# First step of a fused attention and feed-forward kernel: when the first weights are loaded, who assembles the scores, who fills x's gaps, and in what pieces GpSimd works

## The reference

```python
for t in range(S):                       # S = 768
    cur = einsum('bhd,bhe->bhde', u[None] * kt, vt)
    y[:, :, t] = einsum('bhd,bhde->bhe', rt, state + cur)
    state = wt[:, :, :, None] * state + einsum('bhd,bhe->bhde', kt, vt)
x = y.transpose(0, 2, 1, 3).reshape(3072, 384)
h = x @ w_in;  x = where(h > 0, h, exp(min(h, 0)) - 1) @ w_out      # first layer
h = x @ w_in2; x = (h * sigmoid(1.702 * h)) @ w_out2                # second layer
```

## Time and profile before

| | |
|---|---|
| median of 3 runs | 989.51 us (989.06 to 989.93) |
| the profiled execution's own time | 990.9 us |
| its span | 988.7 us |
| PE busy | 943.1 us, 95% of the span |
| PE weight loads busy | 916.1 us, 93% |
| DVE busy | 554.5 us, 56% |
| ACT busy | 457.9 us, 46% |
| POOL busy | 73.0 us, 7% |
| PE in the chain that ended last | 94% |

### The profile page before, as it was taken

The page is one execution under the profiler, slowest core; times in us unless marked ns, Lnnn a source line. Parts: engine busy times, 40 slices in busy tenths (PEclk is TensorE's granted clock), DMA queues, the critical chain, the costliest instruction groups (busy, mean ns, idle before and its releaser), DMA issues.

```text
span 988.7 us, 27078 instructions
## 1 busy us (share of the span) xinstructions
PE 943.1 (95%) x11872; PEld 916.1 (93%) x11872; DVE 554.5 (56%) x910; ACT 457.9 (46%) x875; POOL 73.0 (7%) x66
## 2 busy tenths in 40 slices
PE   3678999999999999999999999999999999999998
PEld 3568999999889999999999999999999999999998
DVE  7899576586676675766853434343433343434333
ACT  3445645636437446455464764333333333333332
POOL 1055000000000000000000542000000000000000
PEclk9979999999999999999999999999999999999999
DMA  7361131221211402212003620000000000000000
GB/s 206 80 170 34 37 94 26 56 51 25 58 50 26 103 3 59 71 26 56 27 2 116 258 81 1 25 1 24 0 18 7 5 19 0 24 1 25 1 25 25
DMA packets 15734, 47.30 MB, mean 48 GB/s; under 512 B 2864, under 2 KB 6832, under 8 KB 15632
## 3 DMA queue, kind: packets, MB, share of 16 engines
q1 hardware_dynamic: 13600, 40.50, 14.7%
q0 software_dynamic: 1552, 4.84, 1.8%
q10 hardware_dynamic: 480, 0.40, 0.2%
HBM read 35.71 MB, written 8.85 MB: 45 GB/s over the span
## 4 chain that ended last, share of the span: by engine, by line
PE 94%; issue 3%; DVE 2%; DMA 1%; ACT 0%; SPq 0%; POOL 0%; DVEq 0%; ACTq 0%; POOLq 0%
PE psum L1214 42%; PE psum L1227 41%; PE psum L1004 4%; PE psum L1114 2%; PE psum L966 1%; PE psum L1109 1%; PE psum L1082 1%; PE psum L1047 1%; PE psum L1040 1%; DMA arena<-w_channels_dram 0%; DVE arena L673 0%; DVE blocks L727 0%; ACT blocks L413 0%; DVE arena L667 0%; PE psum L1013 0%
## 5 line engine op out<-in xcount | busy, mean ns | idle before, releaser
L1214 PE MATMUL psum<-x_hi,w_split 128*128 128x384 f32 x1536 | 395.1, 338 | 0.7 <-issue 0.6
L1227 PE MATMUL psum<-g_hi,w_split 128*128 128x384 f32 x1536 | 393.0, 337 | 0.0
L1214 PEld LDWEIGHTS psum<-x_hi,w_split 128*128 128x128 f32 x1536 | 281.1, 188 | 1.2 <-issue 1.1
L1227 PEld LDWEIGHTS psum<-g_hi,w_split 128*128 128x128 f32 x1536 | 278.5, 189 | 0.4 <-issue 0.3
L1214 PE MATMUL psum<-x_lo,w_split 128*128 128x384 f32 x768 | 263.5, 343 | 5.1 <-DVE x_lo L757 4.1
L1227 PE MATMUL psum<-g_lo,w_split 128*128 128x384 f32 x768 | 262.2, 341 | 0.1
L472 ACT ACTIVATE g_hi<-gate 128x384 fp32r<-128x384 f32 x256 | 134.5, 525 | 178.6 <-DVE gate L776 96.1
L781 DVE TENSOR_TENSOR g_lo<-gate,g_hi 128x384 fp32r<-128x384 f32 x256 | 150.1, 586 | 117.9 <-ACT g_hi L472 117.7
L774 DVE TENSOR_TENSOR gate<-expo,psum 128x384 f32<-128x384 f32 x128 | 70.8, 554 | 162.6 <-ACT expo L468 162.6
L1214 PEld LDWEIGHTS psum<-x_lo,w_split 128*128 128x128 f32 x768 | 144.6, 188 | 6.5 <-issue 4.2
L1227 PEld LDWEIGHTS psum<-g_lo,w_split 128*128 128x128 f32 x768 | 144.9, 189 | 2.9 <-issue 0.6
(11 more groups left out here) (86 smaller groups left out, 458.3 us busy)
## 6 DMA issues: line engine op xcount, KB each, us to landing
v_sb<-v_tokens_dram SPq DMA_DIRECT2D x8, 576.0 KB, 6.2
arena<-w_channels_dram SPq DMA_DIRECT2D x14, 288.0 KB, 5.0
arena<-k_channels_dram SPq DMA_DIRECT2D x14, 288.0 KB, 4.4
arena<-r_channels_dram SPq DMA_DIRECT2D x14, 288.0 KB, 4.9
x_scratch<-x_sb SPq DMA_DIRECT2D x7, 576.0 KB, 3.2
arena<-x_scratch SPq DMA_DIRECT2D x1, 4032.0 KB, 12.5
staging<-weights_dram SPq DMA_DIRECT2D x9, 384.0 KB, 3.6
blocks<-weights_dram SPq DMA_DIRECT2D x9, 384.0 KB, 4.0
```

Source lines behind the costliest of these rows:

```text
L1214: mm = pe.matmul(hidden(f), w_tile(f, lo, m * P), xx, start=n == 0, stop=n == 3 * KT - 1)
L1227: mm = pe.matmul(acc(to, m), w_tile(f, lo, (KT + m) * P), gg, start=f == 0 and n == 0, stop=f == NF - 1 and n == 2)
```

## The change

The change touches the first step and the weights' split.

1. SP no longer issues v, the identity and the five first weight slices behind the inputs. It waits for DVE's updates of the first pair of heads: slices 0, 1 and the identity after level 1, slice 2 after level 2, slice 3 and v after level 3, slice 4 after level 4. The load of the next step's w waits for level 5 of both pairs (before: level 1).
2. DVE does level 1's update of the first pair after two of six products of the tree instead of after all six.
3. The fourth strip of scores is assembled by DVE (`first_assemble`), the other three by ACT. PE's third group of transposes takes bank 0 again and waits for ACT's first copy; the wait for the first pick moves on to the key-value products.
4. Of the six gap DMAs, SP issues two (four before), ACT two as before, POOL two.
5. DVE's low halves: slices 0 and 1 no longer stand between the picks and the states; slice 5 goes to POOL (11 slices there), and slice 4 comes after x's split. ACT's high halves of slices 5 to 15 are issued later, two slices nearer to their use.
6. DVE does the last five products of step 1's tree after the update of level 1, and no longer ahead of the first gate.
7. POOL's low half is four instructions of 192 columns and no longer one of 768.

```diff
@@ turn_banks, gaps_filled @@
-            return (FIRST[0], FIRST[1], FIRST[2]) if is_first(i) else (Z, X, Y)
+            return (FIRST[0], FIRST[1], FIRST[0]) if is_first(i) else (Z, X, Y)
...
                 engine.wait_ge(gap_first, 32)
-                engine.wait_ge(gap_low, 64)
-            else:
-                engine.wait_ge(gap_low, i * 48 + 64)
-                engine.wait_ge(gap_high, i * 48)
+            engine.wait_ge(gap_low, i * 48 + 32)
+            engine.wait_ge(gap_high, i * 48 + 32)
@@ SyncE @@
-                            sp.wait_ge(upd_first[pair], 1)
+                            sp.wait_ge(upd_first[pair], 5)
...
-                        sp.dma_start(x_raw[112:128, 2, :], y3[96:112, 0, :]).then_inc(gap_low, 16)
...
-                    for m in range(KT):
+                    for m in range(2 if is_first(i) else KT):
...
-                sp.dma_start(v_sb[:].rearrange("p c u a e -> p (c u a e)"), v_dram[0]).then_inc(v_in, 16)
-                sp.dma_start(ident[:, :], ident_dram).then_inc(ident_in, 16)
-                for f in range(NW1):
-                    sp.dma_start(w1_raw[f], weights1[f]).then_inc(w1_first[f], 16)
+                for level, fs in ((1, (0, 1)), (2, (2,)), (3, (3,)), (4, (4,))):
+                    sp.wait_ge(upd_first[0], level)
+                    for f in fs:
+                        sp.dma_start(w1_raw[f], weights1[f]).then_inc(w1_first[f], 16)
+                    if level == 1:
+                        sp.dma_start(ident[:, :], ident_dram).then_inc(ident_in, 16)
+                    if level == 3:
+                        sp.dma_start(v_sb[:].rearrange("p c u a e -> p (c u a e)"), v_dram[0]).then_inc(v_in, 16)
@@ GpSimd @@
-                    at = 2 * f * WF
-                    pool.tensor_tensor(w_split[:, at + WF:at + 2 * WF], w1_raw[w1_place(f)],
-                                       w_split[:, at:at + WF].bitcast(F32), ALU.subtract).then_inc(wlo_done, 1)
-
-                for f in range(NW1, 8):
+                    at, n = 2 * f * WF, WF // 4
+                    for z in range(4):
+                        low = pool.tensor_tensor(w_split[:, at + WF + z * n:at + WF + (z + 1) * n],
+                                                 w1_raw[w1_place(f)][:, z * n:(z + 1) * n],
+                                                 w_split[:, at + z * n:at + (z + 1) * n].bitcast(F32), ALU.subtract)
+                    low.then_inc(wlo_done, 1)
+
+                pool.wait_ge(wlo_done, 1)
+                load(5)
+                pool.wait_ge(y3c_first, 1)
+                pool.wait_ge(y3d_first, 1)
+                pool.dma_start(x_raw[48:64, 2, :], y3[32:48, 0, :]).then_inc(gap_high, 16)
+                pool.dma_start(x_raw[112:128, 2, :], y3[96:112, 0, :]).then_inc(gap_high, 16)
+                for f in range(6, 8):
                     pool.wait_ge(wlo_done, f - NW1 + 1)
                     load(f)
-                pool.wait_ge(wlo_done, 6)
-                load(8)
-                for f in range(6, NF):
+                pool.wait_ge(wlo_done, NW1)
+                for f in range(NW1, NF):
                     w1_low(f)
@@ ScalarE @@
-                        after = {2: 10, 3: 11, 4: 12, 5: 13, 6: 14, 7: 15}
+                        after = {2: 8, 3: 9, 4: 10, 5: 11, 6: 12, 7: 13, 8: 14, 9: 15}
...
                     off32(i, 1)
+                    higher(8)
                     whole(g, 9 + s)
+                    higher(9)
...
-                for j in range(4):
+                for j in range(3):
                     assemble(0, j)
-                w1_high(5)
-                w1_high(6)
                 act.wait_ge(y3_first, 2)
...
-                w1_high(7)
                 first_split()
                 for u in range(U):
                     bonus(1, u)
+                w1_high(5)
                 act.wait_ge(wlo_done, NW1)
                 whole(0, 0)
-                w1_high(8)
+                w1_high(6)
                 whole(0, 1)
-                w1_high(9)
+                w1_high(7)
@@ VectorE @@
+                def first_assemble(j):
+
+                    dve.wait_ge(pick_done, N_PICK)
+                    o = 32 * j
+                    t = 32 * (j % 2)
+                    dve.tensor_copy(scores[o:o + 32, :, :, :, t:t + 32].rearrange("p u c a t -> p (u c a) t"),
+                                    diag[o:o + 32, :].rearrange("p (g t) -> p g t", t=32)).then_inc(asm_done, 1)
...
-                for m in range(6):
+                for m in range(2):
                     tree_pair(m, 0)
-                for k in range(1, 3):
-                    grow_pair(k, 0)
+                grow_pair(1, 0)
+                for m in range(2, 6):
+                    tree_pair(m, 0)
+                grow_pair(2, 0)
...
-                for f in range(2):
-                    w1_low(f)
+                first_assemble(3)
                 states(0, 0, 0, range(6))
-                w1_low(2)
+                w1_low(0)
                 dve.wait_ge(y3_first, 2)
                 dve.tensor_copy(*y3_first_view(1)).then_inc(y3d_first, 1)
-                for f in range(3, 5):
+                for f in range(1, 4):
                     w1_low(f)
...
                 first_split()
-                w1_low(5)
-                for m in range(1, 6):
-                    tree(1, m)
+                w1_low(4)
                 gated(0, 0)
...
                 grow_k(1, 1)
+                for m in range(1, 6):
+                    tree(1, m)
                 step(0, 1, 1, 0, 0)
@@ TensorE @@
                         if n == 8:
-                            pe.wait_ge(pick_done, PICKS[1])
+                            pe.wait_ge(kt_done, 1)
...
                     pe.wait_ge(kt_done, i * N_KT + N_KT)
+                    if is_first(i):
+                        pe.wait_ge(pick_done, PICKS[1])
                     pe.sem_inc(level_open, 1)
```

## The result

| | before | after |
|---|---|---|
| median, measured side by side | 990.36 us (18 runs) | 994.44 us (18 runs, 990.9 to 997.7) |
| ratio after / before | | 1.0039, 95% interval 1.0027 to 1.0050 |
| profiled execution, span | 990.9, 988.7 us | 994.93, 992.8 us |
| POOL busy | 73.0 us | 89.5 us |

The change makes the kernel 4 us slower, not 6 us faster: 10 us off, with the wrong sign. Up to 100 us the walk of the prediction is nearly that of the trace. The loss comes right behind it, from 101 to 126 us.

The account below looks back on a forecast made before the run. PE bounds from 400 us on, PE and DVE share 66 to 100 us, and waits through DVE, ACT and DMAs lie ahead. Gains 1.9 + 4.1 = 6.0 us; median 983.5 us, range 979.5 to 988.0.

Parts of the forecast that it names:

- Loads level by level: Start to about 37 us: later weight loads free PE's instruction fetch; 3.06 us gained, 1.2 given back, net 1.9 us.
- The second stop: PE's 0.66 us stop 256 passes after the one near 14 us, read as an instruction wait with DMAs idle.
- the first stop's price: PE's 2.17 us stop near 14 us: DMA traffic was said to delay its instruction block by about 3.2 us.
- Assemble: First step's scores: ACT does three of four strips, so PE's outputs come 0.86 us earlier.
- Gaps: Split of x: two gap DMAs per queue, last landing about 49.4 us; PE's first `up` gains 0.48 us.
- First gate, tree, levels 1 to 4: Step 1: gate follows exp at once, level 1 2.2 us earlier, level 3 only 1.2, level 4 3.3 us.
- POOL in quarters: 66 to 100 us: DVE needs 5.5 us, not 7.9, from level 3 to 4; 4.1 us gained at 100 us.
- POOL starves: Rival, chance 0.06: quarters wait for DVE, slices take 8.9 us, ACT and PE wait for weights; 993.3 us.
- What would show it wrong: PE stopping as long at a later block, or ACT waiting for staging buffers between 65 and 100 us.

Follow-up runs that it names:

- the quarters and the later order: Kernel before, with POOL's low half in four pieces and ACT's high halves of slices 8 to 15 two units later: 984.75 us, 0.9946.
- k held: Changed kernel, with SP holding its load of k until slice 15 has landed: 990.24 us, 1.0004 against the kernel before.
- slice 15 alone moved: Changed kernel, with ACT's high half of slice 15 behind the key copies and slice 10's gate: 988.91 us, 1.0005 against the kernel before.

## Why the prediction was wrong

- **Loads level by level:** right in kind; right in size because two terms that were both too large cancel (3.06 - 1.2 forecast, 2.45 - 0.59 in the trace). 1.9 us forecast, 1.85 in the trace (last pick done at 36.90 and not 38.75 us), 1.8 alone. The second stop, from which the price of the first was taken, was not at idle DMAs: the earlier trace rows shows 22 to 22.5 us, but from 21.0, where the request was put, to 21.5 the DMA engines were busy 0.93 of the time, as this row of the kernel before shows (its last three numbers are clock, DMA share and GB/s):

```profile
21.00:21.50 0.50, 0.50 (x48) 0.50 (x41) 0.50 (x1) 0.00 (x0) 0.00 (x0) 1.00 0.93 184
```

  So the 3.2 us of the first stop's price have no undisturbed row to stand on. The Trainium skill, "Runtime: NRT & Kernel Launch", section "Instruction fetch mechanics", calls such a crossing "mostly hidden"; the 2.17 us that went with the loads say that it isn't under 16 busy DMA engines, and this case's trace disagrees with the page at the next stop too (0.66 us before, 1.25 after).
- **Assemble:** right (0.86 forecast, 0.87 measured on ACT), but not seen in the time of the kernel that has it.
- **Gaps:** wrong in size. I counted queues and let the DMAs land at their old pace (2.5 to 2.9 us in the profile before); with slice loads, r and v around them they take 4.1 to 4.7 us. The split waits 3.02 us, and the first `up` starts at 50.96 us, 0.9 us sooner than before, where 1.9 + 0.48 = 2.4 were forecast.
- **First gate, tree, levels 1 to 4:** right in the mechanism. The gate follows its exp at once, the tree costs what it should. With the 1.9 us of the loads in it the forecast had PE ahead by 4.1 us at level 1, 3.1 at level 3, 5.2 at level 4 and 6.0 at 100 us; the trace has 2.3, 2.6, 4.7, and 5.2 at the transposes (95.04 us). What the gaps took is mostly won back by level 4. Two slips in the working change nothing: 66.8 + 3.9 + 0.8 is 71.5 and not 71.3 us, and the lower bound of the loads' gain is 3.06 - 3.2 = -0.1 and not -0.2 us.
- **The step that failed is "POOL in quarters".** It priced the quarters by what DVE gains and let the 4.1 us at 100 us stand to the end ("Whatever PE gains there it keeps, since PE is dense behind"). That DVE gains is right: with the quarters alone PE is 3.0 us ahead at the transposes (97.22 and not 100.24 us), and the kernel is 4.7 us faster. What was put at nothing is what stands behind them, the wait of ACT for slice 15 with the key copies behind it: 4.05 us of PE standing still at 101 us, 3.4 us of half clock, and about 1.8 us of a second stretch at half clock. What the quarters cost POOL (5.3 us per slice) I had written down only as the rival "POOL starves", with a 0.06 chance, "from 7.2 us per slice on". Its mechanism is the right one: ACT, in order, waits for weights, and PE behind it. Its threshold was wrong for three reasons that the runs show. ACT's high halves stood two units later, so that POOL's later slices began later: load(15) goes out at 86.40 us with the quarters alone, at 97.49 with the quarters and the later order, at 96.29 in the changed kernel. I took 4.4 us for a load; beside k's it took 6.6 (k held: 3.7 us, 1.0004). And I priced PE's stop at its own length, without the stretch at half clock behind it, 3.4 us.
- **What would show it wrong** was named: "ACT is seen waiting for staging buffers between 65 and 100 us". It is, for 1.30 us up to 94.14 and from 97.2 us on. POOL's slices were to stay under 5 us; the longest takes 5.29. The change lists the high halves that move on ACT, and the prediction charges nothing to them. The question that was missing: what stands behind `w1_high(15)` now, and when does its load go out?

The sum of what the runs give: 7.2 us are the places of slices 14 and 15 in ACT's program, 0.9966 remains, 3.4 us of gain where I had forecast 6.0. Of the missing 2.6 us the gaps may be up to 2; the rest is not settled.

## What to carry to other kernels

When an in-order engine gets a wait for a transfer, look at what is queued behind it and put the work that others need first; issuing one such copy behind the three that others need, and another one slice later, was worth 7 us here. Price a helper engine by when its last piece is ready, not only by what it takes from others: quarters gave 4.7 us on the kernel before and nothing in the changed one (1.0039, and 1.0027 with the slice whole). And two large loads issued from different queues within 0.3 us delayed each other here (6.6 us and not 3.7). They met time after time because both waited for the same DVE instruction: look for what two transfers have in common before calling their meeting chance.

## What the runs showed of the hardware

- The same four subtractions of 192 columns on POOL take 2.27 us undisturbed (1.84 us as one of 768) and up to 5.29 us beside DVE, while the worst wait of a `g_lo` shrinks from 1.8 us (2.40 - 0.59) to 0.4 (0.96 - 0.55). The Trainium skill, "SBUF — State Buffer", section "Who interferes with whom", has it that the two exclude each other for the whole instruction; the trace agrees (in the changed kernel a quarter of 0.6 us takes 2.20 us beside an update that takes 2.08), and what a finer cut does here is to move the waiting from DVE to POOL.
- The load of slice 15, 384 KB, takes 3.2 to 3.8 us with no k beside it, 4.1 us when k's two of 288 KB go out 1.04 us behind it, and 6.3 to 6.7 us when they go out 0.31 us behind it, in seven traces (k's take 6.2 us in the changed kernel, 4.1 to 4.8 apart from slice 15). Gap DMAs of 24 KB take 2.9 us on ACT's queue before and 4.7 in the changed kernel.
- After PE had stood for about 4 us ahead of the key-value products, the granted clock fell to 1.2 GHz for some 7 us (stops of 4.05, 4.15 and 3.70 us) or half of that (3.88 us). After stops of 1.10 us or less there it stayed at 2.4 GHz. The stop's length is not all that counts: behind the products with the state the clock fell for 3.4 us more in three of the four kernels with the long stop, after stops of at most 0.82 us; in the kernel with the quarters alone it fell there too, after 0.55 us, and in the one with slice 15 alone moved, where PE stopped 2.24 us ahead of the outputs, it did not.
- The runs of the changed kernel spread over 6.8 us; the other kernels here spread over 3.6 to 9.3 us. A single run can't show any of these effects.
